# Four routing groups, token ranks computed after the first expert's split, fewer warming products, flag read during the last scatter

## The reference

```python
for t in range(S):                                   # attention, per batch and head
    y[t] = r[t] @ (state + outer(u * k[t], v[t]))
    state = w[:, None] * state + outer(k[t], v[t])
expert_idx = argmax(x @ w_gate)                      # one expert per token
gate_w = softmax probability of that expert
for i in range(N):                                   # in token order
    e = expert_idx[i]
    if counts[e] < capacity: disp[e, counts[e]] = x[i]; pos[i] = counts[e]; counts[e] += 1; keep[i] = True
y = relu(disp @ w1) @ w2                             # per expert
out[i] = gate_w[i] * y[expert_idx[i], pos[i]] if keep[i] else 0
h = out @ w_in
result = (h - tanh(h)) @ w_out
```

## Time and profile before

| | us |
|---|---|
| three timed runs | 467.38, 472.07, 473.45 |
| median | 472.07 |
| span of the profiled execution, first to last instruction | 464.8 |
| what lies around the span, by the fastest and the slowest of the three | 2.6 to 8.7 |
| PE busy | 436.0 (94%) |
| DVE, ACT, POOL busy | 248.1, 186.8, 170.0 |

### The profile page before, as it was taken

How to read it: one execution, slowest core, us unless ns; L and a number is a source line. 1 busy time by engine, 2 the same in 40 slices (tenths; PEclk the granted TensorE clock), 3 DMA queues, 4 the chain that set the end, 5 groups by cost and what they waited for, 6 DMA issues and landing times.

```text
span 464.8 us, 9049 instructions
## 1 busy us (share of the span) xinstructions
PE 436.0 (94%) x2993; PEld 422.4 (91%) x2994; DVE 248.1 (53%) x509; ACT 186.8 (40%) x442; POOL 170.0 (37%) x145
## 2 busy tenths in 40 slices
PE   6999999996499999999999998999999999999991
PEld 6888889895399999999999998999999999999991
DVE  8786759876926654654654654524333342525250
ACT  1434324555216566565575575312312231322120
POOL 7575536673804254163263364840200100020002
PEclk9799979998569999999999999999999999999997
DMA  8987867832727856846747745000100000010001
GB/s 233 256 267 241 269 207 211 268 134 89 244 82 226 271 177 220 265 142 216 256 149 231 237 161 169 5 5 2 51 0 0 17 34 0 0 51 0 0 0 56
DMA packets 52317, 63.22 MB, mean 136 GB/s; under 512 B 3712, under 2 KB 48064, under 8 KB 52288
## 3 DMA queue, kind: packets, MB, share of 16 engines
q1 hardware_dynamic: 39408, 52.13, 35.2%
q10 hardware_dynamic: 10912, 5.90, 4.4%
q0 software_dynamic: 1968, 4.83, 2.9%
HBM read 52.71 MB, written 10.13 MB: 135 GB/s over the span
## 4 chain that ended last, share of the span: by engine, by line
PE 83%; DVE 11%; issue 2%; ACT 1%; POOL 0%; DMA 0%; DVEq 0%; POOLq 0%; ACTq 0%
PE ring L967 12%; PE ring L969 12%; PE ring L968 12%; PE pO L1135 7%; PE pO L1136 7%; PE pO L967 5%; PE pO L969 5%; PE pO L968 5%; PE pY L1043 4%; PE pY L1044 3%; PE pA L1018 2%; PE pA L975 2%; DVE owner L847 2%; PE pY L1035 2%; PE pT L1030 1%
## 5 line engine op out<-in xcount | busy, mean ns | idle before, releaser
L426 POOL TENSOR_TENSOR w_lo<-raw_weights,w_hi 128x768 fp32r<-128x768 f32 x40 | 73.3, 1844 | 99.0 <-ACT w_hi L529 99.0
L918 DVE SCALAR_TENSOR_TENSOR minus_tanh<-square,ring 128x384 f32<-128x384 f32 x64 | 35.5, 554 | 99.9 <-ACT square L667 99.9
L529 ACT ACTIVATE w_hi<-raw_weights 128x768 fp32r<-128x768 f32 x80 | 66.3, 847 | 34.7 <-DMA raw_weights<-w 34.7
L667 ACT ACTIVATE square<-ring 128x384 f32<-128x384 f32 x64 | 31.5, 492 | 103.3 <-DVE h_hi L926 59.3
L967 PE MATMUL ring<-yT_hi,w_hi 128*128 x192 | 65.1, 339 | 1.4 <-DVEq L912 1.4
L1135 PE MATMUL pO<-w_hi,h_hi 128*128 128x384 f32 x192 | 65.5, 341 | 0.0
L969 PE MATMUL ring<-yT_hi,w_lo 128*128 x192 | 65.0, 339 | 0.0
L968 PE MATMUL ring<-yT_lo,w_hi 128*128 x192 | 65.0, 338 | 0.0
L1136 PE MATMUL pO<-w_lo,h_hi 128*128 128x384 f32 x192 | 64.9, 338 | 0.0
L507 POOL DMA_INDIRECT out<-out_rows,tok x12 | 11.6, 969 | 126.0 <-ACT out_rows L661 122.8
L967 PE MATMUL pO<-h_hi,w_hi 128*128 128x256 f32 x192 | 54.9, 286 | 0.0
(11 more groups left out here) (154 smaller groups left out, 888.5 us busy)
## 6 DMA issues: line engine op xcount, KB each, us to landing
raw_weights<-w SPq DMA_DIRECT2D x80, 384.0 KB, 4.2
rkT<-rk_by_feature SPq DMA_DIRECT2D x12, 512.0 KB, 5.7
x_by_slot<-x ACTq DMA_DIRECT2D x9, 576.0 KB, 7.9
rkv<-rkv_by_token SPq DMA_DIRECT2D x12, 384.0 KB, 6.2
x_expert<-x_by_slot SPq DMA_DIRECT2D x8, 576.0 KB, 5.0
rkv<-rkv_by_token SPq DMA_DIRECT2D x12, 192.0 KB, 2.5
vb<-v_by_half SPq DMA_DIRECT2D x24, 96.0 KB, 2.7
x_expert<-x_by_slot ACTq DMA_DIRECT2D x1, 576.0 KB, 5.1
```

What stands on the lines that cost most here:

```text
L426: pool.tensor_tensor(lo, unit_raw(2, k), hi.bitcast(F32), ALU.subtract).then_inc(w2_ready, 1)
L529: act.activation(hi, unit_raw(what, k), ACT.Copy).then_inc(w1_hi if what == 1 else w2_hi, 1)
L667: act.activation(sq[:, i % 2, :], ring[i % 4][:, 0:CAP], ACT.Square, scale=THIRD ** 0.5, accum_out=sqsum[:, bass.ds(t * (2 * FC) + i, 1)]) ...
L918: dve.scalar_tensor_tensor(out=nt[:, i % 2, :], in0=sq[:, i % 2, :], scalar=1.0, in1=ring[i % 4][:, 0:CAP], op0=ALU.subtract, op1=ALU.mult ...
```

## The change

1. The routing groups are (0, 4), (4, 4), (8, 2), (10, 2). `route1` of a group runs two steps after the group's last step, `route2`, `positions` and the exponential three steps after. The scatters of a group start four steps after its last step, two a step: rows 0 and 1 at step 7, rows 2 and 3 at step 8, rows 4 and 5 at step 11, the other six after the loop.
2. The running sums of the one-hot rows are one scan with a mask (`carry`) in place of one addition for each step, and one small copy brings the sums of the group before. The one-hot rows lie by expert.
3. On DVE the counting, and of the rank computation the part that PE waits for, stand ahead of the low parts `low(0, 2, 0)` and `low(0, 3, 0)`; the rest of the ranks stands behind the split of `x_expert` and the four low parts of the second expert.
4. PE no longer waits for `rank_ready` ahead of the transposes, and runs 8 and 10 warming products in place of 10 and 22.
5. ACT splits `x_expert` before the four high parts of the second expert (two of them stood ahead of it).
6. POOL's last round of scatters stands outside the loop, and the flag is read between their issue and the wait for their landing.

```diff
-GROUPS = [(0, 5), (5, 5), (10, 2)]
+GROUPS = [(0, 4), (4, 4), (8, 2), (10, 2)]
...
-XS = GS + 5
+XS = 10
...
+        def ended(n):
+            return [g for g, (first, size) in enumerate(GROUPS) if first + size - 1 == n]
+        def dispatched(n):
+            return [i for g in ended(n - 4) + ended(n - 5) for i in range(*GROUP_TOKENS[g])
+                    if (i - GROUP_TOKENS[g][0]) // 2 == n - 4 - (GROUP_TOKENS[g][1] - 1)]
...
@@ gpsimd
                     token_products(n + 1)
-                for i in (2 * (n - GS - 4), 2 * (n - GS - 4) + 1):
-                    if 0 <= i < GS:
-                        scatter(i)
+                for i in dispatched(n):
+                    scatter(i)
                 if n + 1 < STEPS:
                     end_keys(n + 1)
...
-            with pool.Fori(0, TC) as t:
-                rows_out(o_done, o_sc, t, tok3_made, ost_free)
+            with pool.Fori(0, TC - 1) as t:
+                rows_out(o_done, o_sc, t, tok3_made)
+                landed(o_sc, t)
+                pool.sem_inc(ost_free, 1)
+            rows_out(o_done, o_sc, TC - 1, tok3_made)
             pool.wait_ge(flag_ready, 1)
             large = pool.value_load(large_i[0:1, 0:1], min_val=0, max_val=P)
+            landed(o_sc, TC - 1)
...
@@ scalar
-            expo(1)
+            sent = sum(len(dispatched(n)) for n in range(STEPS))
             logit_copy(STEPS - 2)
+            expo(2)
             xt_copy(STEPS - 1)
+            for n in range(sent, 8):
+                scale_x(n)
             high(2, 0, 0, 0)
...
-            high(1, 1, 0, 1)
-            high(1, 1, 1, 1)
             split_x(0, CAP)
-            high(1, 1, 2, 1)
-            high(1, 1, 3, 1)
+            for k in range(4):
+                high(1, 1, k, 1)
...
@@ vector
-                for i in range(m):
-                    link(dve.tensor_tensor(upto[:, i + 1, :], upto[:, i, :], onehot[:, i, :], ALU.add))
+                if g > 0:
+                    link(dve.tensor_copy(expert_major(steps, g)[:, :, 0], upto(g - 1)[:, GROUPS[g - 1][1], :]))
+                width = E * (m + 1)
+                link(dve.tensor_tensor_scan(uptos[:, 0:width], carry[:, int(m < GS), 0:width], steps[:, 0:width], 0.0,
+                                            ALU.mult, ALU.add))
...
@@ tensor
-                if n == GS + 3:
-                    positions(0)
+                for g in ended(n - 3):
+                    positions(g)
...
-            keep_warm(10, ones[:, :], pA0[:, 0, :])
+            keep_warm(8, ones[:, :], pA0[:, 0, :])
             pe.wait_ge(kb_in, 1)
...
-            keep_warm(22, ones[:, :], pA0[:, 0, :])
-            pe.wait_ge(rank_ready, 1)
+            keep_warm(10, ones[:, :], pA0[:, 0, :])
```

More of the change, by code:

```diff
@@ L54 @@
 THIRD = 1.0 / 3.0
+GROUP_TOKENS = [(first, first + size) for first, size in GROUPS]
 SMALL = 7.8e-5
@@ L306, in carries, with expert_major, onehot, upto @@
             return n // C * (C - 1) + min(n % C + 1, C - 1)
+        def ended(n):
[3 more added lines that the diff above has]
+                    if (i - GROUP_TOKENS[g][0]) // 2 == n - 4 - (GROUP_TOKENS[g][1] - 1)]
+        def expert_major(row, g):
+            m = GROUPS[g][1]
+            return row[:, 0:E * (m + 1)].rearrange("p (e i) -> p e i", e=E)
+        def onehot(g):
+            return expert_major(steps, g).rearrange("p e i -> p i e")[:, 1:GROUPS[g][1] + 1]
+        def upto(g):
+            return expert_major(uptos, g).rearrange("p e i -> p i e")
         def place(n):
@@ L498, in _, with rows_out @@
             pool.wait_ge(tok_in, 16)
-            def rows_out(done, scattered, t, made, free):
+            def rows_out(done, scattered, t, made):
                 pool.tensor_copy(tok3[:, :], tok_i[:, bass.ds(t * 3, 3)]).then_inc(made, 1)
@@ L815, in _ @@
                     low(0, 0, 0)
-                if n == GS + 2:
-                    route1(0, rlink)
-                if n == GS + 3:
-                    route2(0, rlink)
-                if n == STEPS - 1:
-                    route1(1, rlink)
+                for g in ended(n - 2):
+                    route1(g, rlink)
+                for g in ended(n - 3):
+                    route2(g, rlink)
             output(STEPS - 1)
-            route2(1, rlink)
+            route2(2, rlink)
             low(0, 1, 0)
-            route1(2, rlink)
-            route2(2, rlink)
-            low(0, 2, 0)
-            low(0, 3, 0)
+            route1(3, rlink)
+            route2(3, rlink)
             link = chained(dve, m_c)
```

89 lines of the change are left out of this document (47 added, 42 removed).

## The result

| | median of the timed runs | lowest to highest | profiled execution | its span |
|---|---|---|---|---|
| before | 472.76 us (4 runs) | 467.38 to 479.42 | the one shown ahead of the prediction | 464.8 |
| changed | 490.43 us (4 runs) | 481.73 to 511.55 | 488.62 us | 486.8 |

The ratio is 1.028 with a 95% interval from 1.018 to 1.038: the change makes the kernel slower, though this interval alone leaves open whether by over 2%. The forecast was 483.5 with a range from 476.5 to 490.0, added up on the earlier median of 472.07. Median against median, the measured time is 6.9 us above the forecast and 0.4 above the range. By the ratio, 1.028 x 472.07 = 485.5, it is 2.0 above the forecast (whose ratio was 1.024) and inside the range. The sign was right.

The account below looks back on a forecast made before the run. The prediction took PE as the bound, busy 436.0 of 464.8 us, with idle and half-clock stretches. It summed +10.5 (attention) +3.0 (clock) -1.2 (to first expert) -0.9 (end) = +11.4 on 472.07, giving 483.5 us, range 476.5 to 490.

Parts of the forecast that it names:

- The stall: Attention step 8: POOL's early scatter waits for the ninth zero transfer, delaying PE 10.4 us, bounds 8.9 to 11.3.
- the section on the attention: Attention steps 7 to 9: scatter wait holds POOL and PE without locking up; 10.5 us late including 0.1 for routing.
- The clock after the stall: Attention steps behind PE's standstill begin at half clock, costing 3.0 us, bounds 0 and 4.5.
- Routing elsewhere: Other routing pieces in attention steps 5, 6, 9 and 10 are hidden in idle time; 0.1 us added.
- The cover at step 6: `route2(0)` (2.05 us) at step 6 hides in 2.23 us of idle time; if not, it costs 0.2 to 0.5.
- Attention to first expert: Between last attention step and first expert: gain of 6.1 or 2.3 us; 1.2 net after what is given back.
- held case: DVE is held by POOL's low parts before the first expert, `x_expert` leaves at about 130.2; gain 2.3 us.
- What is given back: At the first expert: 3.4 us lost at half clock, or 1.8 waiting for DVE's ranks at full clock.
- The end: End of kernel: flag load done while the last rows fly; gain 0.9 us, bounds 0 and 1.
- The second, heavier one: Rival: stall 11.3, clock 4.5, DVE held and clock low at first expert; +16.0, 488.1 us; chance 0.17.
- Not slower: Rival: `x_expert` load leaves at 123.04 as before, gaining 9.5, without a cold clock; +0.1, 472.2 us; chance 0.05.
- no stall: Rival: the ninth transfer is issued or landed early enough, or the change does otherwise than said; 469.2 us; chance 0.03.

Follow-up runs that it names:

- e1: Changed kernel with only the scatters of rows 0 to 3 put back to steps 9 and 10; median 480.6 us.
- e2: Changed kernel, scatters still early, with the nine zero transfers issued in steps 0 to 5 instead of 0 to 8; median 485.6 us.
- the repeat: The changed kernel measured once more, unaltered; median 510.0 us, ratio 1.052 (1.040 to 1.063) to the kernel before.
- e3: Changed kernel with 34 warming products added on PE in step 8 ahead of its state product; median 489.2 us, ratio 1.029.
- e6: The kernel before, unchanged, run for a second trace; median 481.3 us.
- e7: e1 with the ranks on DVE put back ahead of the split of `x_expert`, nothing else; median 474.4 us.
- e9: The kernel of e5 unchanged, with more rounds; median 482.7 us, ratio 0.983 (0.974 to 0.992) to the kernel before.
- e5: Changed kernel with scatters at steps 9 and 10 and the old DVE order, without PE's rank wait, 10 and 10 warming products; median 463.8 us.
- e8: e1 with 34 warming products in place of 10 ahead of the transposes; median 474.7 us, ratio 0.991.

## Why the prediction was right in sign, and short by 2 to 7 us

**The stall: right in mechanism and place, too large.** POOL waited at the first scatter for the ninth zero transfer, PE stood in step 8, nothing locked up, as the section on the attention says. In an undisturbed step (e1, e2) the state product starts 2.65 us after the step's first DVE instruction; in the changed kernel 92.50 - 81.69 = 10.81, in the repeat 84.37 - 73.50 = 10.87. The stall is 8.2 us, and less the 0.8 of routing that left steps 7 and 8 it is 7.4 net, where I had 10.4 with a lower bound of 8.9: outside its bounds. Two causes: the transfer landed at most 6.0 us after its issue, not 8.2, and, a slip of mine, step 8 begins 0.6 earlier once step 7 has no routing, so the transfer is issued earlier too.

**The clock after the stall: the step that failed.** I priced it at 3.0 with bounds 0 and 4.5, from one half-clock stretch of 6.7 us. Steps 7 to 9 grew by 14.82, of which 7.4 is the stall: 7.4 us are the clock, in step 8 19.05 - 7.46 - 8.16 = 3.4 and in step 9 4.07. The 3.4 is borne out by e3. The 4.07 is what the slow products account for in this trace, but a high clock would hardly have given it back: in e3 it was full for the first 9.03 us of that step, and the step took 11.02, held by DVE. I had no term for that. In the repeat steps 8 to 11 took 58.4 against 29.1, so the clock cost some 21 us. The error was to take a stretch's length from a place where the clock came back soon, though the earlier trace rows already held the warning: the second stretch there, from 112.0 to 135.6, lasted 23.6 us. In these runs the cost of the stall was the stall and a stretch behind it of no fixed length. That a stall makes the stretch more likely rests on 10 executions with none under 62 us of half clock, where the kernel before has 20 of 36 under that (one with the stall and warming, e3, had 60); but 62 to 87 also came from the kernel before alone (e6), so the share of luck in any one number is large.

**Luck in the sum.** Stall and clock together were 13.5 in the forecast and 14.8 in the trace, so close only because the stall was taken 3.0 too large and the clock 4.4 too small. The whole forecast was +11.4, and the rows of the table that the change reaches give +17.6.

**Routing elsewhere: a small miss.** The cover at step 6 failed, as the prediction had allowed: at full clock that step took 7.84 us against 7.46, so 0.4, within its 0.2 to 0.5. Step 10 took 8.51 where I had counted `route2` as hidden, step 11 5.70 against 6.44; the net is 0.3, near the 0.1 that I had added.

**Attention to first expert: right, with the held case.** DVE was held by POOL's two low parts, `x_expert` left at 21.76 us after the last output (held case: 130.2 - 106.94 = 23.3), and the first matmul came at 30.48 (held case 30.8). The gain was 2.6, predicted 2.3 for that branch; in the repeat it was 1.5. (The kernel before took 33.08 and, in e6, 32.35.) The Trainium skill (SBUF — State Buffer, section "Who interferes with whom") names conversions among what can contend with GpSimd, if their operands allow a mode that uses both ports. `tail_i` is a conversion with one input and was held, which agrees; no row shows in which mode it ran. The page lets the loser wait for the other's one instruction, 1.8 us, and lets the first to issue win. The rows show otherwise on both: `tail_i` starts at 137.84, POOL's first low part at 138.02, right behind a scatter, and DVE is held 3.78 us over two low parts in a row, as the earlier trace rows showed 7.80 over four. Here the measurement decides.

**What is given back: wrong as an either-or.** I wrote that it is 3.4 at half clock or 1.8 at full clock. The clock was at 0.50 over the transposes, as said, from 150.5 on, but it came back at 157.3, 0.3 us into the expert's first products, where I had half clock for 6.9 us more. Then DVE came late by 2.67 us, and the clock was low again from 164.1, the end of that wait, for 3.4 us: the wait and a shorter stretch of half clock were both paid, 4.2 us by the second expert's transposes. The size of DVE's lateness was short as well: I had summed eight instructions, 2.0 us, and left out the register loads behind them, which the low parts had hidden before. e7 shows that the ranks' place makes the lateness: with them back ahead of the split, 14.4 is 8.9. This term was -1.2 in the sum and measured -2.60 + 4.22 = +1.6.

**The end: -0.9 predicted, about -0.6 measured.** The flag is loaded ahead of the landing, as said, in 762 ns:

```profile
L545 POOLq TENSOR_LOAD <-large_i x1: 762/762/762, 479.1 to 479.1; - x1
```

**The rivals.** The second, heavier one, at 488.1 came nearest to the median, but not by its ingredients: DVE was held, the clock cost more than its 4.5, the stall was 7.4 and not 11.3, and the clock was low at the first expert only for 0.3 us and again behind DVE's lateness. "Not slower" needed `x_expert` to leave as early as before; it left 5.7 us later. The stall was there, so "no stall" falls.

## What to carry to other kernels

A wait that is moved ahead of work in the same queue costs what the last of its signals allows, so list when each of them is issued before moving it; here a second transfer in each of three early steps took the stall out of steps 8 and 9. Behind the stall, look also at what the delayed engine then runs in one go: in e3 POOL's catching up held DVE. Register loads cost nothing here while independent work ran on the engine, and 2.32 us when a chain of dependent small instructions was put in front of them. Where a clock varies from run to run, fit the time against it before judging a median: e2 and e9 would have been misread, and only the rows of one step told what the edit did.

## What the runs showed of the hardware that I had not expected

- The clock can stay at its lower level while PE works without a pause: 19.2 us of 19.2 in the changed kernel, 39.3 of 39.3 in its repeat. When it comes back isn't explained by these runs.
- With the clock full, one expert takes 17.94 us in the kernel before (the same in e6), and 17.0 or 17.6 to 17.7 in the changed one and every variant, in several traces both. PE is busy throughout in both; it runs more products in the same time, 420 against 434 in 50 us:

```profile
225.00:275.00 50.00, 50.00 (x420) 50.00 (x420) 26.00 (x49) 29.72 (x60) 19.63 (x11) 1.00 0.64 210
```

```profile
240.00:290.00 50.00, 50.00 (x434) 50.00 (x433) 27.78 (x52) 31.07 (x64) 20.37 (x12) 1.00 0.69 224
```

  That is worth 3 to 6 us over the experts, and part of why the variants beat the kernel before at equal clock. Nothing in the diff touches those products. The first row is the kernel before, the second the changed one; the cause is open.
- In the dense pair behind the experts it is the other way round. From its first product to PE's last it took 169.9 us in both traces of the kernel before and 168.5 in e5, e7 and e8, all at full clock and without a pause. In every other trace it took 173.6 (the changed kernel) to 175.6 (its repeat), with pauses of 0.4 to 1.1 us with no releaser and a half-clock stretch of 3 to 7 us behind them. This goes neither with the kernel's code alone nor with its data: e5 and e9 are the same kernel, and took 168.5 without a pause and 175.4 with two pauses of 1.06 us and shorter ones. In the experiments the traces without pauses are all from one chip and those with pauses from two others, but the kernel before was never traced on those two. A supply of instructions that comes late would look so too. No run tested either, and the cause is open.
